# Retention of both batches in one turn, on swapped partition halves and four quarters of TensorE

## The chip, the cores and the metric

One NeuronCore of one Trainium2 chip. The metric is the device time of one execution, in microseconds (us). All five engines take part: PE (matmuls), ACT, DVE, POOL (elementwise work) and SP (which issues most of the DMAs).

## The reference

Everything is fp32. A retention (attention with a decay and without softmax) over 2 batches, 8 heads, 576 positions and 64 features a head gives x of 1152 tokens by 512. Then four experts with relu, weighted by normalized probabilities, and a second layer pair with the Mish activation.

```python
scores = (1/8) * q @ k.T                                  # per batch and head, 576 x 576
ret = scores * where(pos_i >= pos_j, gamma_h ** (pos_i - pos_j), 0)
x = (ret @ v).transpose(0, 2, 1, 3).reshape(1152, 512)
p = probs / (probs.sum(-1) + 1e-9)
y = sum(p[:, e:e+1] * (relu(x @ w1[e]) @ w2[e]) for e in range(4))   # 512 -> 1024 -> 512
h = y @ w_in                                              # 512 -> 2048
out = (h * tanh(softplus(h))) @ w_out                     # 2048 -> 512
```

## The kernel before

The retention runs in chunks of 64 positions, 9 for each batch, batch after batch, 18 in all. A chunk lies in a slot of `qkv` (6 slots of 512 KB): partitions 0-63 (`KEYS`) hold v and k by tokens, partitions 64-127 (`FEATS`) hold k and q by features. One turn on PE does three things:
- the scores of the next chunk (L434: k by features times q by features, 8 heads, contraction over 64 partitions 64-127, result on partitions 0-63 of one of three banks) interleaved head by head with the update of the state by this chunk (L438: k times decayed v, contraction over partitions 0-63, result on partitions 64-127, added up in two banks);
- at places given by `AFTER_SCORES` and `AFTER_OUTPUT`, half a tile of the first layer of expert 0 (L480 to L482; three matmuls for each product, since every fp32 operand is split into a high and a low part in fp32r);
- the output of the chunk before (L474): masked scores and state together are one operand over 128 partitions, v and q the other. DVE writes the masked scores over k (L792), so the mask has to wait until the state has been updated; ACT copies the state over k by features of the next slot (L677).

POOL multiplies v by the decay of its key (`v_decay`, L993), two chunks ahead. DVE applies the decay of the row to the output (L807), ACT and DVE split it into high and low part (L683, L813). SP loads chunks and weight blocks of 256 KB (L391, L400) in one order written out by hand. ACT makes the high part of each weight block (L354), POOL the low part (L381); a table `IN_TURN` says in which turn. The job "s" makes the sums of weight quarters that a Strassen-like product of the later stages takes (L368 to L376 on POOL, L350 on ACT).

After the retention PE takes the products of the second layer of stage 0 (`second`, 12 times three matmuls), then stage 2 and so on: 36 stages, in which first-layer products (`product`, P1 to P7) and second-layer products of the stage before alternate. Their order isn't touched. The names for the prediction: JOB "w2" u is the split of block u of the second layer; `second(1, 0)` needs block 4.

Of the kernel before, what the change touches and what calls it, by code (L numbers as in the profile page):

```python
# [13 lines left out]
P = 128  # L14
# [4 lines left out]

CH = 64  # L20
PER_BATCH = SEQ // CH
CHUNKS = BATCH * PER_BATCH
PAIRS = HEADS // 2
MID = SEQ // 2
SLOTS = 6
KEYS, FEATS = slice(0, CH), slice(CH, P)
# [9 lines left out]
PER_BLOCK = TC // CH  # L36
# [8 lines left out]
CONSTS = STEP0 + PER_BATCH * PAIRS


def has_state(c):
    return c % PER_BATCH < PER_BATCH - 1


def states(c):

    return sum(has_state(i) for i in range(c + 1))
# [3 lines left out]
TURNS = CHUNKS + 1  # L58
SCORES = 3
HS = HEADS // 2  # L60
# [3 lines left out]
AFTER_SCORES = {8: (0, 1), 9: (1, 1), 10: (2, 1), 11: (3, 1), 12: (4, 1), 13: (5, 0), 14: (5, 1),  # L64
                15: (6, 0), 16: (6, 1), 17: (7, 0), 18: (7, 1)}
AFTER_OUTPUT = {7: (0, 0), 8: (1, 0), 9: (2, 0), 10: (3, 0), 11: (4, 0)}
HIDDEN_IN = {t: c for c, (t, half) in AFTER_SCORES.items() if half}

ROWS_IN = {0: 4, 1: 5, 6: 6, 7: 7, 8: 8}
# [56 lines left out]
def plan():  # L126
# [46 lines left out]
def build(nc, chunks_in, consts_in, probs_in, weights_in, out):  # L173
    with ExitStack() as ctx:
# [5 lines left out]

        w_hi = sb("w_hi", [P, 2, UNITS, DM], F32R)
# [47 lines left out]
        mask = consts[KEYS, MASK0:ROW0]  # L229
# [4 lines left out]
        ps_s = [banks[i][KEYS, :].rearrange("p (h c) -> p h c", h=HEADS) for i in range(SCORES)]  # L234
        ps_state = [banks[i][FEATS, 0:HS * DH].rearrange("p (h c) -> p h c", h=HS) for i in range(2)]
        ps_o = banks[3][:, 0:PAIRS * CH].rearrange("p (h c) -> p h c", h=PAIRS)
# [10 lines left out]
        s_st = sem("s_st")  # L247
        s_o = sem("s_o")
# [28 lines left out]
        def by_keys(c, which):  # L277
            return qkv[KEYS, c % SLOTS, which]

        def by_feats(c, which):  # L280
            return qkv[FEATS, c % SLOTS, which]

        def landed(c):
            return 16 * (c // SLOTS + 1)

        def x_chunk(c):

            at = slice(CH * (c % PER_BLOCK), CH * (c % PER_BLOCK + 1))
            if c < PER_BLOCK:
                return x_tmp[:, c % 2], xa_hi[:, :, at], xa_lo[:, :, at]  # L290
            full = xf[:, :, CH * (c - PER_BLOCK):CH * (c - PER_BLOCK + 1)]
            if c < 2 * PER_BLOCK:
                return full, xb_hi[:, 0:KT, at], xb_lo[:, 0:KT, at]
            return full[:, KH:], xb_hi[:, KT:, at], xb_lo[:, KT:, at]
# [11 lines left out]
        def x_full(e, i):  # L306

            if e == 0:
                return (xs_a, xs_b)[i // 2][:, i % 2]
            return (x2_b[:, 0:KH], x2_c[:, KH:], x2_c[:, 0:KH], x2_b[:, KH:])[i]  # L310

# [18 lines left out]
        def weight_free(act, job):  # L330
# [56 lines left out]
        def _(sp):  # L387
            def load_chunk(c):
                if c >= SLOTS:
                    sp.wait_ge(s_o, c - SLOTS + 1)  # L390
                sp.dma_start(qkv[:, c % SLOTS], chunks_in[c]).then_inc(s_slot[c % SLOTS], 16)  # L391

            def chunk_there(c):
                sp.wait_ge(s_slot[c % SLOTS], landed(c))
# [9 lines left out]
            sp.dma_start(consts[KEYS, 0:ROW0], consts_in[KEYS, 0:ROW0]).then_inc(s_const, 16)  # L404
            load_chunk(1)

            for c in range(2, 6):
                if c > 2:
                    chunk_there(c - 3)
                load_chunk(c)  # L410
            for u in range(UNITS):
                chunk_there(3 + u)
                load_weights(u)
                chunk_there(4 + u)
                load_chunk(6 + u)
            for c in range(6 + UNITS, CHUNKS):
                chunk_there(c - 3)
                load_chunk(c)
                load_weights(UNITS + c - 6 - UNITS)
            sp.dma_start(ident[:, :], consts_in[:, CONSTS:]).then_inc(s_id, 16)  # L420
            for r in range(UNITS + CHUNKS - 6 - UNITS, len(LOADS)):
                load_weights(r)
            by_rows = out.rearrange("(g p) d -> p g d", p=P)
            sp.wait_ge(s_af, read(EXPERTS - 1, TT - 1))
            sp.dma_start(by_rows[:, 0:TT, :], acc_sb[:, 0:TT, :]).then_inc(s_out, 16)
            for g in range(TT, TPP):
                sp.wait_ge(s_af, read(EXPERTS - 1, g))
                sp.dma_start(by_rows[:, g, :], acc_sb[:, g, :]).then_inc(s_out, 16)
            sp.wait_ge(s_out, 16 * (1 + TPP - TT))

        @block.tensor
        def _(pe):
            def scores_head(c, h):
# [28 lines left out]
            def output(c):  # L462
# [7 lines left out]
                if c > 0:  # L470
                    pe.wait_ge(s_xt, c)
# [584 lines left out]
```

## Time and profile before

| | |
|---|---|
| median of 3 runs | 634.28 us (629.97 to 635.52) |
| the profiled execution | 630.54 us, span 628.8 us |
| instructions | 9476 |
| granted clock of PE over the span | 1.00 |
| DMA | 50.41 MB, mean 80 GB/s |

The span runs from the first to the last instruction of the profile. A page shows busy times by engine, a chain of work that ended last, groups of instructions, and DMA issues; the other views cut the same trace into stretches, or list it in order of time. A name in a row such as bank<-qkv is what was written and what was read.

### The profile page before, as it was taken

The page shows a single profiled execution, that of the slowest core. Times are in us where ns is not written, and L with a number is a line of the kernel's source. Part 1 is how long each engine was busy: PE and PEld are TensorE (multiplying, and loading weights), DVE is VectorE, ACT ScalarE, POOL GpSimd, SP SyncE. Part 2 cuts the span into 40 slices and gives each one's busy share as a digit, 9 for nine tenths or more (in the row PEclk, how much of TensorE's full clock was granted, in tenths as well). Part 3 has the DMA queues.
Part 4 walks back from the last instruction along what each step waited for, and adds up shares of the span by engine and source line. Part 5 has one row for each costly group of instructions (what it writes and reads, how often), then busy time and mean ns, then how long its engine had stood idle before and what let it go on. Part 6 is the DMA issues. An engine that isn't in the chain of part 4 may idle for free.

```text
span 628.8 us, 9476 instructions
## 1 busy us (share of the span) xinstructions
PE 620.6 (99%) x3764; PEld 553.7 (88%) x3765; DVE 243.5 (39%) x388; ACT 238.0 (38%) x459; POOL 284.4 (45%) x239
## 2 busy tenths in 40 slices
PE   8999999999999999999999999999999999999997
PEld 5788899998999999899999899989979999999996
DVE  5756743333143333143323143335564333314324
ACT  3555433332223432223432223435544455334432
POOL 4759535543435542535543535532553544443300
PEclk9999999999999999999999999999999999999999
DMA  8954312222112322102321202321100232201002
GB/s 275 339 177 158 111 34 68 100 88 64 51 35 67 101 84 67 51 34 67 101 84 56 62 35 67 101 67 47 55 34 34 68 116 85 68 0 52 1 0 100
DMA packets 25146, 50.41 MB, mean 80 GB/s; under 512 B 2896, under 2 KB 3216, under 8 KB 25104
## 3 DMA queue, kind: packets, MB, share of 16 engines
q1 hardware_dynamic: 24816, 49.66, 24.2%
q8 instruction: 30, 0.49, 0.3%
q10 hardware_dynamic: 288, 0.17, 0.1%
q14 instruction: 12, 0.10, 0.0%
HBM read 47.45 MB, written 2.36 MB: 79 GB/s over the span
## 4 chain that ended last, share of the span: by engine, by line
PE 95%; DVE 3%; ACT 1%; issue 0%; POOL 0%; DVEq 0%; ACTq 0%; POOLq 0%
PE bank L480 30%; PE bank L482 30%; PE bank L481 30%; PE bank L434 2%; PE bank L474 2%; DVE xt L896 1%; PE bank L612 1%; PE bank L605 1%; PE bank L438 1%; DVE acc_sb L866 0%; DVE acc_sb L870 0%; ACT h_hi L708 0%; DVE h_lo L826 0%; DVE acc_sb L975 0%; ACT h_act L691 0%
## 5 line engine op out<-in xcount | busy, mean ns | idle before, releaser
L381 POOL TENSOR_TENSOR w_lo<-w_raw,w_hi 128x512 fp32r<-128x512 f32 x96 | 128.8, 1356 | 151.0 <-ACT w_hi L354 151.0
L482 PE MATMUL bank<-w_hi,h_lo 128*128 128x512 f32 x432 | 169.9, 393 | 0.0
L481 PE MATMUL bank<-w_lo,h_hi 128*128 128x512 f32 x432 | 169.5, 392 | 0.0
L480 PE MATMUL bank<-w_hi,h_hi 128*128 128x512 f32 x432 | 169.0, 391 | 0.0
L376 POOL TENSOR_TENSOR ws<-ws_f,ws 128x1024 fp32r<-128x1024 f32 x24 | 57.9, 2412 | 150.4 <-ACT ws L350 150.4
L853 DVE TENSOR_TENSOR h_act<-part,bank 128x384 f32<-128x384 f32 x96 | 52.8, 550 | 179.4 <-PE bank L482 179.4
L482 PEld LDWEIGHTS bank<-w_hi,h_lo 128*128 128x128 f32 x432 | 81.0, 188 | 17.5
L481 PEld LDWEIGHTS bank<-w_lo,h_hi 128*128 128x128 f32 x432 | 81.0, 188 | 9.8
L480 PEld LDWEIGHTS bank<-w_hi,h_hi 128*128 128x128 f32 x432 | 81.1, 188 | 9.6
L703 ACT ACTIVATE h_hi<-h_act 128x384 fp32r<-128x384 f32 x64 | 33.6, 526 | 104.8 <-DVE h_act L853 104.8
L713 ACT ACTIVATE part<-bank 128x384 f32<-128x384 f32 x72 | 35.2, 489 | 82.9 <-PE bank L482 82.2
L480 PE MATMUL bank<-xa_hi,w_hi 128*128 128x384 f32 x192 | 66.6, 347 | 0.0
L482 PE MATMUL bank<-xa_hi,w_lo 128*128 128x384 f32 x192 | 64.7, 337 | 0.0
L481 PE MATMUL bank<-xa_lo,w_hi 128*128 128x384 f32 x192 | 64.5, 336 | 0.0
L819 DVE SCALAR_TENSOR_TENSOR h_lo<-h_act,h_hi 128x384 fp32r<-128x384 f32 x64 | 47.3, 739 | 35.5 <-ACT h_hi L703 35.5
L826 DVE TENSOR_TENSOR h_lo<-h_act,h_hi 128x384 fp32r<-128x384 f32 x48 | 32.5, 677 | 69.2 <-ACT h_hi L708 69.1
L354 ACT ACTIVATE w_hi<-w_raw 128x512 fp32r<-128x512 f32 x96 | 57.3, 618 | 0.0
L480 PE MATMUL bank<-xt,ws 128*128 128x384 f32 x144 | 48.6, 337 | 1.3 <-DVE xt L896 1.2
L481 PE MATMUL bank<-xt,ws 128*128 128x384 f32 x144 | 48.6, 337 | 0.0
L482 PE MATMUL bank<-xt,ws 128*128 128x384 f32 x144 | 48.5, 337 | 0.0
L819 DVE SCALAR_TENSOR_TENSOR h_lo<-bank,h_hi 128x384 fp32r<-128x384 f32 x32 | 17.7, 554 | 67.7 <-ACT h_hi L694 67.7
L694 ACT ACTIVATE h_hi<-bank 128x384 fp32r<-128x384 f32 x32 | 15.7, 491 | 71.2 <-PE bank L482 71.2
(87 smaller groups left out, 916.0 us busy)
## 6 DMA issues: line engine op xcount, KB each, us to landing
w_raw<-in_weights SPq DMA_DIRECT2D x144, 256.0 KB, 2.7
qkv<-in_chunks SPq DMA_DIRECT2D x18, 512.0 KB, 4.9
out<-acc_sb SPq DMA_DIRECT2D x6, 256.0 KB, 2.0
out<-acc_sb SPq DMA_DIRECT2D x1, 768.0 KB, 5.3
consts<-in_consts ACTq DMA_DIRECT2D x1, 146.0 KB, 3.8
ident<-in_consts SPq DMA_DIRECT2D x1, 64.0 KB, 4.0
consts<-in_consts SPq DMA_DIRECT2D x1, 34.0 KB, 4.0
p_nat<-in_probs ACTq DMA_DIRECT2D x1, 18.0 KB, 3.9
```

The source lines that it names most:

```text
L354: act.activation(w_hi[:, int(kind == "w2"), x], w_raw[:, r % RAW], ACT.Copy).then_inc(s_wh, 1)
L376: pool.tensor_tensor(w_sum(x)[:, 1], ws_f[:, :], w_sum(x)[:, 0].bitcast(F32), ALU.subtract)\
L381: pool.tensor_tensor(w_lo[:, layer, x], w_raw[:, r % RAW], w_hi[:, layer, x].bitcast(F32), ALU.subtract).then_inc(s_wl, 1)
L480: pe.matmul(out, w[0], x[0], start=first, stop=False, **more)
L481: pe.matmul(out, w[0], x[1], start=False, stop=False, **more)
L482: return pe.matmul(out, w[1], x[0], start=False, stop=last, **more)
L694: act.activation(h_hi[:, tile_slot(s, i)], banks[6 + i % 2][:, 0:TC], ACT.Relu).then_inc(s_hh, 1)
L703: act.activation(h_hi[:, tile_slot(s, i)], h_act[:, i % 2], ACT.Relu).then_inc(s_hh, 1)
L713: act.activation(part[:, i], banks[6][:, 0:TC], ACT.Copy).then_inc(s_pt, 1)
L819: dve.scalar_tensor_tensor(h_lo[:, slot], full, 0.0, h_hi[:, slot].bitcast(F32), ALU.max, ALU.subtract).then_inc(s_hl, 1)
L826: dve.tensor_tensor(h_lo[:, slot], h_act[:, i % 2], h_hi[:, slot].bitcast(F32), ALU.subtract)\
L853: dve.tensor_tensor(h_act[:, i % 2], part[:, kept], banks[bank][:, 0:TC], op).then_inc(s_cc, 1)
```

## The change

One turn now takes the same chunk of both batches, so there are 9 turns instead of 18 and `CH` stays 64. The two batches lie on swapped halves: batch 0 has its tokens on partitions 0-63 (`UPPER`) and its features on 64-127 (`LOWER`), batch 1 the other way. So scores of batch 0, scores of batch 1, state of batch 0 and state of batch 1 use four different quarters of the array. A slot has five columns (Y1, X0, X1, Z, Y0). The masked scores go to column Y of the batch's token half, which holds nothing loaded, and not over k, which is Z: the mask no longer waits for the state. Each slot is loaded by two transfers, one of 64 partitions for columns 0 to 3 and one of 64 partitions for columns 1 to 4. There are four slots of 1 MB; the fourth (`last_slot`) lies where `w_hi` of the second layer lies later, so its splits from block 3 on wait for the output of turn 7 (`FREE_UNITS`). Scores have two banks, the state one, the output two (before one). Tiles of the first layer are no longer cut in halves (`AHEAD`, `BEHIND`). Row decays are a ring of four instead of eight tables. The jobs of weights are spread over the turns anew; on ACT those of the last turn come behind its `first_hi`. The output is stored by two transfers, 64 partitions each, from SP (batch 0) and from ACT (batch 1).

```diff
+AHEAD = {4: 1, 5: 2, 6: 4, 7: 5, 8: 7}
+BEHIND = {3: 0, 5: 3, 7: 6}
+ROWS = 4
+ROWS_IN = {3: 5, 4: 6, 5: 7, 6: 8}
+LOW_AT_ONCE = (PER_BLOCK - 1, CHUNKS - 1)
...
     for u in range(UNITS):
-        add(IN_TURN, 5 + u, "w1", 0, u)
+        add(IN_TURN, 2 + (u + 1) // 2, "w1", 0, u)
     for u in range(3):
-        add(IN_TURN, 12 + u, "w2", 0, u)
-    add(IN_TURN, 15, "s", 0, 0)
-    for u in range(3, 6):
-        add(IN_TURN, 13 + u, "w2", 0, u)
+        add(IN_TURN, 6 + (u + 1) // 2, "w2", 0, u)
+    add(IN_TURN, 8, "w2", 0, 3)
+    add(IN_TURN, 8, "s", 0, 0)
+    for u in range(4, 6):
+        add(IN_TURN, 8, "w2", 0, u)
...
+            elif kind == "w2" and x >= FREE_UNITS:
+                act.wait_ge(s_o, CHUNKS - 1)
...
+            def load_chunk(t):
+                if t >= SLOTS:
+                    sp.wait_ge(s_o, t - SLOTS + 1)
+                sp.dma_start(slot(t)[UPPER, 0:4], chunks_in[t, UPPER]).then_inc(s_slot[t % SLOTS], 16)
+                sp.dma_start(slot(t)[LOWER, 1:5], chunks_in[t, LOWER]).then_inc(s_slot[t % SLOTS], 16)
...
+            for t in range(2, SLOTS):
+                chunk_there(t - 2)
+                load_chunk(t)
+            for t in range(SLOTS, CHUNKS):
+                chunk_there(t - 2)
+                for r in range(2 * (t - SLOTS), 2 * (t - SLOTS) + 2):
+                    load_weights(r)
+                load_chunk(t)
...
+            def scores_head(t, b, h):
+                return pe.matmul(ps_s[t % 2][FEAT[b], h], part_of(t, FEAT[b], X[b])[:, h],
+                                 part_of(t, FEAT[b], Y[b])[:, h], start=True, stop=True)
...
+            def scores_and_state(t):
+
+                n = t + 1
+                pe.wait_ge(s_slot[n % SLOTS], landed(n))
+                if n >= 2:
+                    pe.wait_ge(s_sm, BATCH * (n - 1))
+                pe.wait_ge(s_vd, BATCH * n)
+                if t > 0:
+                    pe.wait_ge(s_st, BATCH * t)
+                for h in range(HEADS):
+                    for b in range(BATCH):
+                        mm = scores_head(n, b, h)
+                    if h == HEADS - 1:
+                        mm.then_inc(s_sc, 1)
+                    for b in range(BATCH):
+                        mm = state_head(t, b, h)
+                mm.then_inc(s_kv, 1)
...
+            def first_output():
+
+                pe.wait_ge(s_vd, BATCH)
+                pe.wait_ge(s_sm, BATCH)
+                for b in range(BATCH):
+                    if b > 0:
+                        pe.wait_ge(s_of, 1)
+                    for h in range(HEADS):
+                        mm = output_head(0, b, h, TOK[b])
+                    mm.then_inc(s_o if b else s_of, 1)
+
+            def output(t):
+
+                pe.wait_ge(s_vd, BATCH * (t + 1))
+                pe.wait_ge(s_sm, BATCH * (t + 1))
+                pe.wait_ge(s_st, BATCH * t)
+                if t >= 2:
+                    pe.wait_ge(s_xt, t - 1)
                 for hp in range(PAIRS):
+                    for b in range(BATCH):
+                        for x in range(2):
+                            mm = output_head(t, b, 2 * hp + x, slice(0, P))
                 mm.then_inc(s_o, 1)
...
+            scores(0)
+            keep_warm(8)
+            for t in range(CHUNKS):
+                if t + 1 < CHUNKS:
+                    scores_and_state(t)
+                if t in AHEAD:
+                    plain_tile(AHEAD[t])
+                if t == 0:
+                    keep_warm(3)
+                    first_output()
+                else:
+                    output(t)
+                if t in BEHIND:
+                    plain_tile(BEHIND[t])
...
+            for t in range(CHUNKS):
+                if t + 1 < CHUNKS:
+                    state_copy(t)
+                if t in AHEAD:
+                    plain_hi(*divmod(AHEAD[t], ITEMS))
+                if t + 1 < CHUNKS:
+                    for job in IN_TURN.get(t, ()):
                         job_hi(act, job)
+                first_hi(t)
+                if t in BEHIND:
+                    plain_hi(*divmod(BEHIND[t], ITEMS))
+            for job in IN_TURN[CHUNKS - 1]:
+                job_hi(act, job)
...
+            def masked(t):
+
+                dve.wait_ge(s_sc, t + 1)
+                for b in range(BATCH):
+                    dve.tensor_tensor(part_of(t, TOK[b], Y[b]), ps_s[t % 2][FEAT[b]],
+                                      mask[FEAT[b]].unsqueeze(1).broadcast_to([CH, HEADS, CH]), ALU.mult).then_inc(s_sm, 1)
...
+            for t in range(CHUNKS):
+                if t + 2 < CHUNKS:
+                    v_decay(t + 2)
+                    pool.wait_ge(s_vd, BATCH * (t + 3))
+                for job in IN_TURN.get(t, ()):
                     job_lo(pool, job)
```

## Rows read from the trace of the kernel before

**Rows 1.** The page, part 1 (busy time) and part 4 (chain, shares by engine).

```profile
PE 620.6 (99%) x3764; PEld 553.7 (88%) x3765; DVE 243.5 (39%) x388; ACT 238.0 (38%) x459; POOL 284.4 (45%) x239
PE 95%; DVE 3%; ACT 1%; issue 0%; POOL 0%; DVEq 0%; ACTq 0%; POOLq 0%
```

**Rows 2.** Busy time in one stretch, the retention.

```profile
core 0: us, PE busy (x) PEld busy (x) DVE busy (x) ACT busy (x) POOL busy (x), PEclk, DMA share, GB/s
7.66:60.80 53.14, 51.01 (x917) 43.88 (x918) 34.28 (x64) 28.55 (x71) 36.96 (x33) 1.00 0.70 241
```

**Rows 3.** The same view, two stretches of 10 us.

```profile
10.00:20.00 10.00, 9.41 (x263) 8.47 (x259) 7.36 (x15) 5.15 (x15) 5.89 (x5) 1.00 0.92 314
20.00:30.00 10.00, 8.62 (x137) 7.39 (x136) 8.54 (x14) 5.31 (x13) 7.27 (x7) 1.00 0.96 342
```

**Rows 4.** The chain that ended last, by time: start us, us, what.

```profile
17.14 0.24 PE bank L434
...
18.29 0.62 PE bank L474 x16
...
20.32 1.38 issue
...
28.20 0.37 PE bank L480
28.57 0.18 PE bank L481
```

**Rows 5.** The timeline of PE at the retention's end: start us, us, instruction.

```profile
59.74 0.69 PE L474 MATMUL bank<-qkv 128*64 128x64 f32 x16
...
68.65 0.33 PE L480 MATMUL bank<-xb_hi,w_hi 128*128 128x384 f32 x1
...
69.72 0.39 PE L480 MATMUL bank<-w_hi,h_hi 128*128 128x512 f32 x1
```

**Rows 6.** The timeline of PE where blocks of two kinds overlap.

```profile
10.36 0.22 PE L474 MATMUL bank<-qkv 64*64 64x64 f32 x1
10.36 0.22 PE L438 MATMUL bank<-qkv 64*64 64x64 f32 x1
10.42 0.22 PE L434 MATMUL bank<-qkv 64*64 64x64 f32 x1
10.42 0.22 PE L474 MATMUL bank<-qkv 64*64 64x64 f32 x1
```

**Rows 7.** The page, part 6: DMA issues, KB each, us to landing.

```profile
w_raw<-in_weights SPq DMA_DIRECT2D x144, 256.0 KB, 2.7
qkv<-in_chunks SPq DMA_DIRECT2D x18, 512.0 KB, 4.9
```

**Rows 8.** The timeline of POOL: start us, us, instruction, idle before.

```profile
8.59 1.04 POOL L993 TENSOR_TENSOR qkv<-qkv,consts 64x512 f32<-64x512 f32 x1 [0.23 <-DMA qkv<-in_chunks]
9.86 1.04 POOL L993 TENSOR_TENSOR qkv<-qkv,consts 64x512 f32<-64x512 f32 x1 [0.23 <-DMA qkv<-in_chunks]
...
20.79 1.27 POOL L381 TENSOR_TENSOR w_lo<-w_raw,w_hi 128x512 fp32r<-128x512 f32 x1 [1.08 <-ACT w_hi L354]
...
54.59 0.73 POOL L368 TENSOR_TENSOR ws_f<-w_raw 128x256 f32<-128x256 f32 x1
...
58.84 2.39 POOL L376 TENSOR_TENSOR ws<-ws_f,ws 128x1024 fp32r<-128x1024 f32 x1 [1.23 <-ACT ws L350]
61.19 4.61 POOL L381 TENSOR_TENSOR w_lo<-w_raw,w_hi 128x512 fp32r<-128x512 f32 x3
```

**Rows 9.** The timeline of ACT.

```profile
8.95 0.65 ACT L677 ACTIVATE qkv<-bank 64x256 f32<-64x256 f32 x2 [6.93 <-PE bank L438]
...
57.64 1.06 ACT L350 ACTIVATE ws<-ws_f 128x1024 fp32r<-128x1024 f32 x1
```

**Rows 10.** The timeline of DVE.

```profile
8.98 0.68 DVE L792 TENSOR_TENSOR qkv<-bank,consts 64x512 f32<-64x512 f32 x1 [1.60 <-PE bank L438]
...
62.60 2.05 DVE L930 TENSOR_TENSOR xs_a<-xf 128x768 f32<-128x768 f32 x1
```

More of the change, by code:

```diff
@@ L35 @@
 KH = KT // 2
-PER_BLOCK = TC // CH
+PER_BLOCK = TC // P
 RAW = 8
 WARM = 9
-MASK0 = PER_BATCH * HEADS
+FREE_UNITS = 3
+MASK0 = CHUNKS * HEADS
 ROW0 = MASK0 + CH
 STEP0 = ROW0 + PAIRS * CH
[L45 to L69, printed above, removed]
+CONSTS = STEP0 + CHUNKS * PAIRS
+AHEAD = {4: 1, 5: 2, 6: 4, 7: 5, 8: 7}
[3 more added lines that the diff above has]
+LOW_AT_ONCE = (PER_BLOCK - 1, CHUNKS - 1)
 STAGES = 6
@@ L275, in build, with slot, part_of, landed @@
         s_out = sem("s_out")
[L277 to L292, printed above, removed]
+        def slot(t):
+            return last_slot if t % SLOTS == SLOTS - 1 else qkv[:, t % SLOTS]
+        def part_of(t, half, column):
+            return slot(t)[half, column]
+        def landed(t):
+            return 32 * (t // SLOTS + 1)
+        def x_chunk(t):
+            at = slice(P * (t % PER_BLOCK), P * (t % PER_BLOCK + 1))
+            if t < PER_BLOCK:
+                return x_tmp[:, t % 2], xa_hi[:, :, at], xa_lo[:, :, at]
+            full = xf[:, :, P * (t - PER_BLOCK):P * (t - PER_BLOCK + 1)]
+            if t < 2 * PER_BLOCK:
                 return full, xb_hi[:, 0:KT, at], xb_lo[:, 0:KT, at]
@@ L403, in _ @@
             load_chunk(0)
-            sp.dma_start(consts[KEYS, 0:ROW0], consts_in[KEYS, 0:ROW0]).then_inc(s_const, 16)
+            sp.dma_start(consts[:, 0:ROW0], consts_in[:, 0:ROW0]).then_inc(s_const, 16)
             load_chunk(1)
[L407 to L415, printed above, removed]
@@ new lines, in state_head, with scores @@
+            def state_head(t, b, h):
+                return pe.matmul(ps_state[FEAT[b], h], part_of(t, TOK[b], Z)[:, h], part_of(t, TOK[b], X[b])[:, h],
+                                 start=(t == 0 and h == 0), stop=True, skip_group_check=True)
+            def scores(t):
+                pe.wait_ge(s_slot[t % SLOTS], landed(t))
+                for h in range(HEADS):
+                    for b in range(BATCH):
+                        mm = scores_head(t, b, h)
+                mm.then_inc(s_sc, 1)
@@ L472, in output @@
+            def output(t):
[4 more added lines that the diff above has]
+                    pe.wait_ge(s_xt, t - 1)
                 for hp in range(PAIRS):
-                    for x in range(2):
-                        mm = pe.matmul(ps_o[DH * x:DH * (x + 1), hp], qkv[rows, c % SLOTS, 0, 2 * hp + x],
-                                       qkv[rows, c % SLOTS, 1, 2 * hp + x], start=True, stop=True)
+                    for b in range(BATCH):
+                        for x in range(2):
+                            mm = output_head(t, b, 2 * hp + x, slice(0, P))
@@ L907, in _ @@
             dve.wait_ge(s_rows, 16)
-            for i in range(1, 4):
+            for i in range(1, ROWS + 1):
                 rows(i)
```

260 lines of the change are left out of this document (106 added, 154 removed).

## The prediction, made before the changed kernel ran

> **What bounds the kernel now.** The page comes first. PE is busy 99% of the span and 95% of the chain that ended last is PE [rows 1]. So a change to retention is worth only what it takes out of PE's own order of work, or puts into it as waiting. The second view is the stretch of the retention, 7.66 to 60.80 us [rows 2]: PE is busy 51.01 of 53.14 us at full clock (1.00, so the upper of its two levels, 2.4 GHz), DVE 34.3, ACT 28.6, POOL 37.0, and the DMA engines 0.70. PE bounds it, and next is not an engine but the DMA: from 10 to 20 us its engines are busy 0.92 at 314 GB/s, from 20 to 30 us 0.96 at 342 GB/s [rows 3]. In these 20 us PE and the loads are nearly level. One can see that in the one long stall of PE, 1.38 us at 20.32 [rows 4]. Whatever makes PE quicker there will meet the loads.
>
> The third view is the chain in detail [rows 4]. A scores-and-state block takes 1.15 us (17.14 to 18.29), after a product 1.1. An output block of one chunk takes 0.62. A product of the first layer opens with 0.37 and then takes 0.175 for each further matmul, so half a tile (6 matmuls) is 0.37 + 5 x 0.175 = 1.24. The sum over the stretch is 17 x 1.1 + 18 x 0.62 + 16 x 1.24 = 18.7 + 11.2 + 19.8 = 49.7, and 0.6 of keep-warm products and 1.4 of stall make 51.7 of the 52.8 us up to the end of the last output at 60.4 [rows 5].
>
> **The change part by part: PE.** Each fp32 head product is two passes. In the trace of PE two passes in the same quarter start 58 ns apart (0.06 in the rows), and passes of two other quarters or lines start beside them: L474, L438 and L434 within the same 0.06 [rows 6]. So three quarters at once run at the pace of one. The new block holds scores and state of both batches, 64 passes over four quarters, 16 deep as now. If the fourth quarter is as free as the third, it costs 1.1 us, for two chunks instead of one. If PE starts passes no faster than these three in 58 ns, it costs 64 x 19.4 = 1.24 plus the 0.2 of filling; at the pace of the common two-wide stretches, 64 x 29 ns = 1.9 plus 0.2. I take 1.1, since the three-wide row is nearest, and keep 2.0 as the other end. Outputs are K=128 products on two column halves before and after: 16 passes in 0.62, so 32 passes in 0.62 + 16 x 0.028 = 1.1. The first output runs each batch by itself with a wait between, 2 x 0.62 = 1.3. Products are no longer cut in halves: 0.37 + 11 x 0.175 = 2.3 a tile. PE's new sum is 8 x 1.1 + 8 x 1.1 + 1.3 + 8 x 2.3 + 0.6 = 38 us against 51.7. By PE alone the change would gain about 14 us.
>
> Here a rule of the Trainium skill speaks against the change. "TensorE: Matmul & The Clock Gate" (section "Wait — 56ns, not 53.3ns?") says that starts of matmuls never come closer than about 25 ns however small they are. By it a block of 64 passes would be an estimated 1.6 + 0.2 us; by the rows, where three starts fit into 58 ns, the floor doesn't hold between quarters, and the sum stays.
>
> **DMA: where most of the gain goes.** The bytes are the same: 18 x 512 KB of chunks [rows 7], now 9 x 1 MB. But PE wants them sooner. Slot 0 and 1 together are the bytes of the first four chunks, and the fourth is there at 9.86, when POOL's decay of it starts [rows 8]. Today PE's first scores-and-state block starts at 7.66 with two chunks there [rows 2]; it will start at 9.9. Then each slot of 1.05 MB needs 3.4 us at 314 GB/s, and from slot 4 on two weight blocks of 256 KB go ahead of each [rows 7]: 1.57 MB, 4.6 us at 342 GB/s. The slots land at 9.9 (slot 1), 13.4, 16.7, 21.3, 25.9, 30.5, 35.1 and 39.7 (slot 8). None waits for a free slot: the load of t waits for the output of t-3, which is earlier.
>
> POOL stands between the loads and the first tiles: v_decay(t+2) is queued ahead of the splits of weights of turn t. A decay of a chunk is 1.04 us, now two a turn, 2.1; a split is 1.27 [rows 8]. Tile 0 (after output 3) needs the split that is queued behind the decay of slot 4: 21.3 + 2.1 + 1.3 = 24.7. Tile 1 needs the one behind the decay of slot 5: 25.9 + 2.1 + 1.3 = 29.3.
>
> **The turns added up.** Block 0 9.9 to 11.0, keep-warm and first output to 12.9. Block 1 waits for slot 2: 13.4, output to 15.6. Block 2 16.7, output to 18.9. Block 3 21.3, output to 23.5. Tile 0 24.7 to 27.0, block 4 to 28.1. Tile 1 29.3 to 31.6, output 32.7. From here PE doesn't wait: block 5, tile 2, output, tile 3 (1.1 + 2.3 + 1.1 + 2.3) to 39.5; block 6, tile 4, output to 44.0; block 7 starts 5 us behind slot 8, tile 5, output, tiles 6 and 7, output to 54.2. Before, it is 60.4. So 6.2 us are gained, and 7 to 8 us of PE's saving are lost to loads and POOL in the first turns.
>
> ACT and DVE have room in this. The state is copied in two pieces of twice the width: 0.65 for the pair now [rows 9], an estimated 1.1 after, against the 1.1 of the output that PE does meanwhile (up to 0.2 a turn in t = 5 to 8 if it isn't covered; only turns without a tile behind the output would show it, and there PE waits for the load). The mask costs DVE 0.68 a chunk as before [rows 10], for the turn after next. Separate places for masked scores take away the mask's wait for the state; nothing waited long for that before, and I cost it at nothing. The four row tables instead of eight and the double output bank too.
>
> **What comes behind the retention.** Here the change moves an order. The split of w2 3, the first weight sums s0 and the splits of w2 4 and 5 now stand behind the last first_hi on ACT, because w2 from 3 on lies where the last slot was. Before, s0 was begun at 54.59, six us before the retention's end, and w2 4 and 5 were done soon after it [rows 8]. Now, counted from the end of the last output: decayed 0.7, first_hi to 1.2, w2 3 on ACT to 1.8 and on POOL to 3.1; four sums of 0.73 (two DVE operations of 2.05 us beside them [rows 10] slow POOL: the three splits there took 4.61 instead of 3.8 [rows 8]) to 6.6; ACT's copy of the sums 1.06 [rows 9] to 7.7; the low part 2.39 to 10.2; w2 4 to 11.6. PE wants it when the 12 products of the second layer (8.3 us) and P1 (1.07) are through, 9.36 after the end of the output [rows 5]. So a new stall of 2.2 us; with nothing slowed it is 1.5, with all of POOL slowed by a fifth 4. Later stages have slack: the next weight sums are needed 20 us on. The output in two halves on two queues sends the same bytes; the last transfer of 128 KB instead of 256 lands no later. I cost it at 0 (bounds -0.3 to +0.5).
>
> Sum: -6.2 + 2.2 = -4.0 us. The profiled execution took 630.54 us (span 628.8), so 626.5 by its measure. The median of the runs is 634.28, 3.7 above it, so the forecast is **630.3 us**, 0.994 of before.
>
> **The rivals.** *Transfers to half of the partitions are slow.* Every load of a chunk is cut into one transfer to partitions 0-63 and one to 64-127. All loads of size in the trace go to 128 partitions, so its price isn't shown. One end is the full rate. For the other: chunks three and four land 1.26 us apart [rows 8], 415 GB/s; if that is a rate that all partitions together allow and half of them allow half, a slot takes 5.0 us, with weights 6.6. Then slot 1 lands at 13.5 and slot 8 at 56.6, and block 7, tile 5, output, tiles 6 and 7 and output (10.2 us) end at 66.8: 6.4 later than before, plus 2.2, +8.6 us, 642.9. It decides from a rate of chunk bytes below 262 GB/s (slot 8 at 48.0). For it speaks that the transfers of one slot run one behind the other; against it that several are in flight and may fill each other's gaps, which would leave it between.
> The Trainium skill, "SBUF — State Buffer" (sections "Door 1: The DMA port swizzle" and "Can I just issue two DMAs to hit both halves?"), says that partitions 0-63 reach only half of the ports, and that two transfers to the two halves serialize, only 6% better than one. By its 218 GB/s the estimate would be +6.3 us. No row here shows it.
>
> *The four quarters don't run at once.* Blocks of 2.0 us: in t = 4 to 7 nothing hides the 0.9, +3.6; 633.9 and no gain.
>
> *No stall behind the retention.* If POOL gets through in time or the loads come earlier than I count them (10% faster loads are 1.5 us at tile 1), it is -6 to -8: 627.5.
>
> **How the numbers follow.** A measurement of this kernel can't tell less than about 1% (6.3 us) from no change. The forecast has 0.44, with its own bounds from 626 to 634: 0.05 of it under 628, the rest same. Slow half transfers 0.33, 635 to 643: 0.21 slower by over 1%, 0.12 same. No overlap of quarters 0.08, all same. No stall 0.15, 0.11 faster. Together faster 0.16, same 0.63, slower 0.21. The range holds the forecast and most of both sides, 625 to 643.
>
> **What the profile would show.** The timeline of PE: blocks of 64 passes of 1.1 us, or 2.0. The waits: POOL's qkv for DMA, with slot 8 there near 40, or near 55. The DMA share in the first 30 us stays at 0.9 and over in all cases, but the GB/s stay at 330 or fall to about 210. PE idle for w_lo of the second layer some 9 us behind the retention. The clock stays 1.00: if the waits of up to 2.4 us in turns 1 to 3 bring it down to 1.2 GHz, the blocks double in length there, yet mostly inside waits for loads. The forecast is wrong if PE waits for slots 6 to 8, or if the last output ends before 52 or after 57.

## The result, and the profile after

The changed kernel takes 653.76 us (median of 4 runs, 652.6 to 654.02), the one before 633.07 (4 runs, 629.97 to 635.52): ratio 1.033, with an interval of 1.029 to 1.036. It is slower, by about 21 us. The profiled execution has a span of 652.1 us against 628.8, so 23.3 us are to be found in the two traces.

The page of the changed kernel, parts 1 (busy time), 4 (shares of the chain that ended last) and 6 (DMA issues):

```profile
PE 621.4 (95%) x3768; PEld 554.8 (85%) x3768; DVE 244.4 (37%) x370; ACT 235.1 (36%) x434; POOL 288.7 (44%) x239
...
PE 84%; DMA 9%; DVE 2%; POOL 2%; issue 1%; ACT 1%; SPq 1%; POOLq 0%
...
qkv<-in_chunks SPq DMA_DIRECT2D x14, 512.0 KB, 10.1
out<-acc_sb SPq DMA_DIRECT2D x6, 128.0 KB, 2.4
out<-acc_sb ACTq DMA_DIRECT2D x6, 128.0 KB, 2.9
```

Beside [rows 1]: PE's share of the chain fell from 95% to 84%, and DMA now has 9%. A transfer of 512 KB of a chunk takes 10.1 us from issue to landing, against 4.9 [rows 7].

The same kernel's busy time in stretches (stretch and length in us; then busy us and instructions of PE, PEld, DVE, ACT, POOL; the granted clock of PE; the mean busy share of the DMA engines; GB/s):

```profile
5.00:15.00 10.00, 5.73 (x105) 3.61 (x104) 2.81 (x6) 0.00 (x0) 3.02 (x3) 0.83 1.04 223
15.00:45.00 30.00, 20.23 (x423) 17.78 (x413) 16.08 (x21) 10.48 (x18) 13.66 (x13) 0.74 1.03 231
65.00:70.00 5.00, 5.00 (x32) 4.56 (x34) 0.96 (x2) 0.96 (x3) 1.65 (x2) 0.50 0.36 108
```

The first two lines are the result in short: they are the stretches in which the slots are loaded. The DMA engines are as busy as in [rows 3] (1.03 against 0.92 and 0.96), but move 223 and 231 GB/s instead of 314 and 342. A share of 1.0 looks like a full pipe; only the GB/s beside it show that it isn't. PE is busy two thirds of the time from 15 to 45 us, at a clock between its levels (0.74).

The timeline of POOL shows when slots land: before each decay of v shown here it stood idle, and the load ended the idle time (in brackets).

```profile
14.05 2.15 POOL L1026 TENSOR_TENSOR qkv<-qkv,consts 64x512 f32<-64x512 f32 x2 [2.71 <-DMA qkv<-in_chunks]
18.91 2.15 POOL L1026 TENSOR_TENSOR qkv<-qkv,consts 64x512 f32<-64x512 f32 x2 [2.70 <-DMA qkv<-in_chunks]
...
54.24 2.15 POOL L1026 TENSOR_TENSOR last_slot<-last_slot,consts 64x512 f32<-64x512 f32 x2 [2.41 <-DMA last_slot<-in_chunks]
...
61.74 2.15 POOL L1026 TENSOR_TENSOR qkv<-qkv,consts 64x512 f32<-64x512 f32 x2 [2.73 <-DMA qkv<-in_chunks]
...
77.93 1.87 POOL L393 TENSOR_TENSOR w_lo<-w_raw,w_hi 128x512 fp32r<-128x512 f32 x1 [5.28 <-ACT w_hi L366]
79.76 1.46 POOL L380 TENSOR_TENSOR ws_f<-w_raw 128x256 f32<-128x256 f32 x1
...
84.13 0.75 POOL L385 TENSOR_TENSOR ws_f<-w_raw,ws_f 128x256 f32<-128x256 f32 x1
86.11 2.36 POOL L388 TENSOR_TENSOR ws<-ws_f,ws 128x1024 fp32r<-128x1024 f32 x1 [1.23 <-ACT ws L362]
88.43 7.86 POOL L393 TENSOR_TENSOR w_lo<-w_raw,w_hi 128x512 fp32r<-128x512 f32 x4
```

Slot 1 is there at 14.05, slot 2 at 18.91 and slot 8 at 61.74. Between slot 1 and 2 it is 4.86 us for 1.05 MB, 216 GB/s; between slot 7 and 8 it is 7.50 us for 1.57 MB with its weight blocks, 210 GB/s. So the blocks of weights, transfers to all 128 partitions, go no faster when they stand between half transfers.

The timeline of PE, around slot 8 and behind the retention:

```profile
61.72 0.27 PE L441 MATMUL bank<-qkv 64*64 64x64 f32 x2 [1.93 <-DMA qkv<-in_chunks]
61.73 0.27 PE L445 MATMUL bank<-last_slot 64*64 64x64 f32 x2
...
61.88 0.22 PE L441 MATMUL bank<-qkv 64*64 64x64 f32 x2
61.89 0.23 PE L445 MATMUL bank<-last_slot 64*64 64x64 f32 x2
61.94 0.23 PE L441 MATMUL bank<-qkv 64*64 64x64 f32 x2
61.95 0.23 PE L445 MATMUL bank<-last_slot 64*64 64x64 f32 x2
...
62.64 0.23 PE L441 MATMUL bank<-qkv 64*64 64x64 f32 x2
...
64.82 0.66 PE L505 MATMUL bank<-xa_hi,w_hi 128*128 128x384 f32 x1 [1.94 <-issue]
...
74.92 1.15 PE L476 MATMUL bank<-qkv 128*64 128x64 f32 x32
...
90.47 0.71 PE L505 MATMUL bank<-w_hi,h_hi 128*128 128x512 f32 x1 [4.95 <-POOL w_lo L393]
```

The four quarters do what the change says: L441 and L445 start two passes each (x2), and the next four start 58 ns later, where [rows 6] has three. The block of 64 passes for two chunks runs from 61.72 to 62.88, in 1.16 us. An output of 32 passes takes 1.15. What is gained there is lost again in PE's waits for the loads, 12.1 us in all up to the retention's end (the kernel before has none).

Where the 23.3 us went:
- The last output ends at 76.0 instead of 60.4 [rows 5]: +15.6. Slot 8 comes at 61.7, and the rest takes 14.3 us.
- PE waits 4.95 us for block 4 of the second layer, a wait that the kernel before hasn't.
- Behind that wait PE runs at the lower clock for some microseconds (0.65 from 90 to 92 us, its matmuls 0.43 us apart instead of 0.23), +1.8 (stage 2's first matmul of P6 begins at 95.96 instead of 73.53, 22.4 us later, and 15.6 + 5.0 of these are in the two points above).
- The end: from DVE's last add to the end of the span 3.4 us instead of 2.5, +0.9.

### The profile page after: what moved, and what is told of

Its sections match the earlier page's. It is cut to its first block, busy times and chain, and to the rows that moved or that the text cites. A ratio compares the mean times of both kernels' runs of the same rounds, so it can differ in the third digit from the quotient of the medians.

```text
span 652.1 us, 9388 instructions
## 1 busy us (share of the span) xinstructions
PE 621.4 (95%) x3768; PEld 554.8 (85%) x3768; DVE 244.4 (37%) x370; ACT 235.1 (36%) x434; POOL 288.7 (44%) x239
## 4 chain that ended last, share of the span: by engine, by line
PE 84%; DMA 9%; DVE 2%; POOL 2%; issue 1%; ACT 1%; SPq 1%; POOLq 0%
PE bank L506 28%; PE bank L507 28%; PE bank L505 28%; DMA qkv<-in_chunks 9%; POOL w_lo L393 1%; DVE xt L922 1%; PE bank L628 1%; SPq L403 0%; POOL ws L388 0%; SPq L413 0%; DVE acc_sb L892 0%; DVE acc_sb L896 0%; DVE h_lo L852 0%; DVE acc_sb L1004 0%; POOL ws_f L381 0%
## 5 line engine op out<-in xcount | busy, mean ns | idle before, releaser
L393 POOL TENSOR_TENSOR w_lo<-w_raw,w_hi 128x512 fp32r<-128x512 f32 x96 | 131.7, 1388 | 144.0 <-ACT w_hi L366 143.6
L507 PEld LDWEIGHTS bank<-w_hi,h_lo 128*128 128x128 f32 x432 | 81.3, 188 | 17.6
L507 PE MATMUL bank<-xa_hi,w_lo 128*128 128x384 f32 x192 | 66.2, 345 | 0.0
L506 PE MATMUL bank<-xa_lo,w_hi 128*128 128x384 f32 x192 | 66.0, 344 | 0.0
## 6 DMA issues: line engine op xcount, KB each, us to landing
qkv<-in_chunks SPq DMA_DIRECT2D x14, 512.0 KB, 10.1
last_slot<-in_chunks SPq DMA_DIRECT2D x4, 512.0 KB, 10.2
```

Of the source, the lines that this page charges most:

```text
L393: pool.tensor_tensor(w_lo[:, layer, x], w_raw[:, r % RAW], w_hi[:, layer, x].bitcast(F32), ALU.subtract).then_inc(s_wl, 1)
L506: pe.matmul(out, w[0], x[1], start=False, stop=False, **more)
L507: return pe.matmul(out, w[1], x[0], start=False, stop=last, **more)
```

## The experiments

Unless it says otherwise, an experiment changes one thing in the kernel before or in the changed kernel ("after"). Ratios are to the kernel before on the same chip, with their 95% interval.

**1. The kernel before with its chunks cut into halves by partitions.**

```diff
-sp.dma_start(qkv[:, c % SLOTS], chunks_in[c])
+sp.dma_start(qkv[KEYS, c % SLOTS], chunks_in[c, KEYS])      # 0-63
+sp.dma_start(qkv[FEATS, c % SLOTS], chunks_in[c, FEATS])    # 64-127
```

> The kernel before, with every 512 KB load of a chunk cut into a transfer to partitions 0-63 and one to 64-127; nothing else. Theory (a transfer to half of the partitions runs at about 215 GB/s): a chunk takes 2.4 us to load instead of 1.5, with a weight block 3.2 to 3.8. The turns without a product (1.8 us) wait for it, those with a tile (4.2 us) don't: 5 x 0.6 + 3 x 1.6, some 8 us slower, 6 to 10, and 210 to 240 GB/s in the first 25 us. Rival (the number of transfers or their issue costs it): the same loss as in the run cut by columns. Rival (layout of slots, chain of waits or array of the changed kernel costs it): no change, 0 to 1 us.

Measured: 637.45 us against 632.52, ratio 1.007 (1.005 to 1.010). The same bytes and the same order, and 4.9 us more. Window, and the timeline of POOL:

```profile
3.00:15.00 12.00, 11.13 (x142) 6.84 (x140) 3.94 (x11) 1.72 (x5) 4.14 (x4) 1.00 1.05 235
```

```profile
10.86 1.04 POOL L994 TENSOR_TENSOR qkv<-qkv,consts 64x512 f32<-64x512 f32 x1 [1.27 <-DMA qkv<-in_chunks]
13.16 1.04 POOL L994 TENSOR_TENSOR qkv<-qkv,consts 64x512 f32<-64x512 f32 x1 [1.26 <-DMA qkv<-in_chunks]
```

A chunk takes 2.3 us (10.86 to 13.16) instead of the 1.27 of [rows 8], 228 GB/s, with the DMA engines at 1.05. The price was expected too high, at 8 us (6 to 10): the kernel before wants a chunk only every 2.9 us on average, and PE's waits for chunks add up to 2.9 us.

**2. The same with two transfers cut by columns**, each to all 128 partitions.

```diff
+for w in range(2):
+    sp.dma_start(qkv[:, c % SLOTS, w], chunks_in[c, :, w])
```

> The kernel before, with every load of a chunk cut into two transfers of 256 KB that both go to all 128 partitions (v or k by features, then k or q). Theory: no change, within 1 us, and 310 to 340 GB/s in the first 25 us. Rival (number of transfers): as slow as the run cut by partition halves.

Measured: 633.67 against 632.52, 1.002 (0.999 to 1.005): no difference. Window of this kernel:

```profile
5.00:10.00 5.00, 5.00 (x32) 2.96 (x33) 0.67 (x3) 0.00 (x0) 3.01 (x3) 1.00 0.97 341
```

Twice the transfers, half as large, at 341 GB/s. From 10 to 15 us it is 232 GB/s, but there the DMA engines are busy only 0.70 of the time, so that isn't a low rate of the transfers. So neither the number nor the size of the transfers is at fault.

**3. The changed kernel with one transfer a slot**, to all partitions. A slot has five columns of which each half needs four, so the fifth is sent as zeros: 1.31 MB instead of 1.05.

```diff
-sp.dma_start(slot(t)[UPPER, 0:4], chunks_in[t, UPPER])
-sp.dma_start(slot(t)[LOWER, 1:5], chunks_in[t, LOWER])
+sp.dma_start(slot(t)[:, :], chunks_in[t])
```

> The changed kernel, with each slot loaded by one transfer to 128 partitions of all five columns. It carries a column of zeros in each half that nobody reads: 1.31 MB a slot instead of 1.05. Theory: at 320 to 340 GB/s a slot takes 3.9 us, with weights 5.5: slot 1 near 12, slot 8 near 47 instead of 61.7; last output near 58 instead of 76, and some 15 to 18 us faster than the changed kernel in spite of 25% more bytes (636 to 639). The wait for the second layer's w2 4 (5 us) stays. Rival (the array or the waits of the turn hold it up, not the loads): not over 3 us faster, or slower by the added bytes.

Measured: 636.13 against 632.52, 1.004 (1.002 to 1.006); 17.6 us less than the changed kernel's median, with a quarter more bytes. Its windows, and its timeline of PE:

```profile
5.00:15.00 10.00, 7.49 (x207) 5.17 (x208) 7.10 (x14) 1.81 (x3) 5.50 (x6) 1.00 0.99 395
15.00:45.00 30.00, 23.92 (x532) 21.74 (x533) 18.84 (x28) 15.10 (x27) 19.93 (x18) 0.89 0.94 346
```

```profile
25.18 0.37 PE L440 MATMUL bank<-qkv 64*64 64x64 f32 x2 [3.52 <-DMA qkv<-in_chunks]
...
56.55 1.15 PE L475 MATMUL bank<-qkv 128*64 128x64 f32 x32
...
72.10 0.80 PE L504 MATMUL bank<-w_hi,h_hi 128*128 128x512 f32 x1 [4.95 <-POOL w_lo L393]
```

POOL begins the decay of slot 8 at 45.86 instead of 61.74 (it comes to it from other work, so the slot is there by then at the latest), and the last output ends at 57.7, before the 60.4 of [rows 5]. Yet the kernel isn't faster: the wait for w2 4 (the split of block 4 of the second layer) stands unchanged, 4.95 us. Loads cost the change its gain, and the order of POOL's jobs costs it the rest.

**4. The changed kernel with the lower halves issued by ACT**, the upper ones by SP, so that two queues work side by side.

```diff
 sp.dma_start(slot(t)[UPPER, 0:4], chunks_in[t, UPPER])
-sp.dma_start(slot(t)[LOWER, 1:5], chunks_in[t, LOWER])
+# on ACT, for t < 4 at the start, else behind first_hi(t - 4)
+act.dma_start(slot(t)[LOWER, 1:5], chunks_in[t, LOWER])
```

> The changed kernel, with the half transfers to partitions 64-127 issued by ACT instead of SP, so that both halves are in flight on two queues at the same time. Theory A (the two queues' transfers mix on the DMA engines and so reach all partitions at once): over 300 GB/s, as fast as with one transfer, 12 us or more faster than the changed kernel. Theory B (the halves hinder each other as much from two queues): within 2 us of the changed kernel, at 215 to 230 GB/s.

Measured: 652.81 against 632.52, 1.031 (1.026 to 1.035), as the changed kernel. Window of this kernel:

```profile
10.00:15.00 5.00, 5.00 (x60) 2.86 (x62) 1.38 (x2) 0.00 (x0) 3.25 (x4) 1.00 1.02 231
```

Still 231 GB/s, and slot 8 at 61.73. Two queues gain nothing over one. This agrees with the Trainium skill, "SBUF — State Buffer" (section "Can I just issue two DMAs to hit both halves?"), which says that transfers issued from several engines run on the same DMA engines, and that two transfers to the two halves serialize.

**5. One transfer a slot, and the first weight sums s0 a turn earlier** (in turn 7, ahead of the splits of w2 1 and 2).

```diff
-add(IN_TURN, 8, "s", 0, 0)
+add(IN_TURN, 7, "s", 0, 0)    # w2 0 to turn 6, w2 1 and 2 behind s0
```

> The kernel with one transfer a slot, with the weight sums s0 moved in the table of jobs from turn 8 to turn 7, ahead of the splits of w2 1 and 2 (so on POOL they come before the retention's end and not behind the last first_hi). Theory (the order of jobs makes the wait of PE for w2 4 behind the retention): the wait of 5.0 us goes, and with it the half clock behind it (1.8 us): 6 to 7 us faster than with one transfer alone, 629 to 631. Rival (POOL is full there, whatever the order): another split or the sums are late in its place, the wait stays over 3 us.

Measured: 628.58 against 631.87, 0.995 (0.993 to 0.998). By the ratios that is 0.9 points (5.6 us) below 3, where 6 to 7 us were expected. The wait for w2 4 is gone, with the last output at 58.4, 0.7 us later than in 3. The view of waits of this kernel, for PE (engine, line, releaser: us in total, times, longest):

```profile
PE bank L441 <- DMA qkv<-in_chunks: 5.0, 3, 3.1
```

**6 and 7. What makes a half slow: 64 partitions, or these 64?** The kernel before with three transfers a chunk: once 0-31, 32-95, 96-127, once 0-31, 32-63, 64-127.

```diff
+for rows in (slice(0, 32), slice(32, 96), slice(96, 128)):    # 6
+for rows in (slice(0, 32), slice(32, 64), slice(64, 128)):    # 7
+    sp.dma_start(qkv[rows, c % SLOTS], chunks_in[c, rows])
```

> The kernel before, with each load of a chunk cut into three transfers: partitions 0-31, 32-95 and 96-127. Theory A (what counts is whether a transfer has partitions of both halves, below and from 64): the middle transfer, half of the bytes, runs at the full rate, the outer two at 215 GB/s: 2.0 us a chunk, 260 GB/s in the first 15 us. Theory B (64 or 32 partitions are slow as such, few rows for 16 DMA engines): no faster than with 0-31, 32-63, 64-127, about 215 to 240 GB/s.

> The kernel before, with the same three sizes cut otherwise: partitions 0-31, 32-63 and 64-127, so that no transfer has partitions of both halves. Both theories: 2.4 us a chunk, 215 to 240 GB/s, as the run cut in halves. It stands beside the run with 0-31, 32-95, 96-127.

Measured: 638.19 (1.010, 1.007 to 1.014) and 638.09 (1.010, 1.006 to 1.013) against 631.87. Windows, first of the kernel with 32-95, then of the other:

```profile
3.00:15.00 12.00, 10.37 (x148) 6.73 (x148) 4.97 (x12) 1.72 (x5) 4.15 (x4) 0.86 1.00 225
```

```profile
3.00:15.00 12.00, 11.44 (x154) 7.15 (x154) 4.72 (x14) 1.93 (x6) 4.14 (x4) 1.00 1.04 234
```

A chunk takes 2.44 us with the middle piece in one and 2.29 without. If a transfer that takes partitions of both halves ran at the full rate, as the theory of the halves has it, the first would be at 2.0. So this pair speaks against that theory, or else the two outer pieces of 32 partitions, one in each half, cost more than their bytes. The pair can't tell which; 9, 13 and 14 look at it in other ways.

**8. The kernel before with its stores in two halves**, from SP and from ACT, as the change has them.

```diff
-sp.dma_start(out, acc_sb)
+sp.dma_start(by_rows[KEYS, ...], acc_sb[KEYS, ...])
+act.dma_start(by_rows[FEATS, ...], acc_sb[FEATS, ...])
```

> The kernel before, with each store of the result cut into partitions 0-63 from SP and 64-127 from ACT, as in the changed kernel; nothing else. Theory (the split of the store costs the 0.9 us that the tail of the changed kernel is longer, from the last DVE row to the end of the span): 0.9 us more, the tail 3.4 instead of 2.5 us. Rival (the store's rows lie apart in DRAM in the changed kernel, and that costs it): tail 2.5 as before.

Measured: 633.56 against 631.87, 1.002 (1.000 to 1.004). The page, part 6, and the timeline of DVE of this kernel:

```profile
out<-acc_sb ACTq DMA_DIRECT2D x6, 128.0 KB, 2.9
```

```profile
624.23 2.05 DVE L872 TENSOR_TENSOR acc_sb<-bank,acc_sb 128x512 f32<-128x512 f32 x3 [2.03 <-PE bank L482]
```

The last add ends at 626.3 as before, and the span at 629.7 instead of 628.8. The tail of 3.4 us is that of the changed kernel: the 0.9 us come from the store. In the times this size can't be told from nothing.

**9. The kernel before with its chunks cut into even and odd partitions**: 64 partitions a transfer, but spread over all 128.

```diff
+for i in range(2):
+    sp.dma_start(qkv[i::2, c % SLOTS], chunks_in[c, i::2])
```

> The kernel before, with each load of a chunk cut into its even and its odd partitions (64 each, spread over both halves). Theory A (a transfer that takes one half of the partitions is slow because of which half): full rate, 310 to 340 GB/s in the first 15 us, 1.5 us a chunk and within 2 us of the kernel before. Theory B (any transfer to 64 partitions is slow): 215 to 240 GB/s, 2.4 us a chunk, some 5 us slower. The run with 32-95 spoke for B.

Measured: 632.86 against 632.74, 1.000 (0.997 to 1.002). Window of this kernel:

```profile
3.00:15.00 12.00, 11.62 (x205) 8.05 (x204) 6.60 (x14) 2.89 (x9) 5.57 (x6) 1.00 0.92 305
```

305 GB/s where the halves have 235 in the same stretch, and a chunk every 1.3 us. The same bytes in two transfers of 64 partitions each: what is slow is not any 64 partitions. The 64 of one half are.

**10. The changed kernel with only s0 a turn earlier**, its half transfers kept.

> The changed kernel as it is (half transfers), with the sums s0 moved from turn 8 to turn 7, ahead of the splits of w2 1 and 2. Theory: the wait of 5.0 us for w2 4 and the half clock behind it go here too, 5 to 7 us faster than the changed kernel, 646 to 648; the rest, over 13 us, is the loads'. Rival (the wait only shows once the loads are quick): no change.

Measured: 644.28 against 632.74, 1.017 (1.013 to 1.021), 9.5 us less than the changed kernel, where 5 to 7 were expected. The wait of 5.0 and the lower clock behind it (1.8) are gone, as counted. What wasn't counted is that the last output ends at 74.1, 1.9 earlier (slot 8 lands 1.1 earlier, at 60.64; no run shows why): together 8.7 (the spans differ by 8.3).

**11. The kernel of 5 without the loads of turns 4 to 8**: POOL and PE use what lies in the slots, so the results of these turns are not the reference's. It shows what faster loads of these turns could give at most.

```diff
+if t >= SLOTS:
+    return    # in load_chunk
```

> The kernel with one transfer a slot and the sums early, in which the loads of turns 4 to 8 are left out: the four slots are loaded once and used again, so the result isn't the reference's; POOL waits for the output that read the slot. It shows the turns without their loads. Theory (four quarters and fewer turns save PE about 14 us, and loads eat it): the last output ends near 48 to 50 instead of 58, 8 to 10 us faster than the kernel with the sums early. Rival (the turn itself, its chain of decay, split, mask and state copy, is what lasts): not over 3 us faster.

Measured: 625.29 against 632.74, 0.987 (0.982 to 0.992). By the ratios that is 0.8 points (5 us) below the kernel of 5; 8 to 10 us were expected. Timeline of PE of this kernel:

```profile
19.51 0.92 PE L475 MATMUL bank<-qkv 128*64 128x64 f32 x23 [3.55 <-issue]
...
53.95 1.15 PE L475 MATMUL bank<-qkv 128*64 128x64 f32 x32
```

From 19.5 on PE waits only once more (0.57 us at 27.20, for DVE), with its clock at 0.66 from 20 to 25 us, and the last output ends at 55.1, where 48 to 50 was expected. That is 0.9 us later than the 54.2 that the prediction gave for loads at full rate. The first four slots and all blocks of weights are still loaded here, and the wait of 3.55 us lies among them, so it isn't shown what loads without any price would give. Without those of turns 4 to 8 the change gains 1.3%.

**12. The kernel of 5 with the load of slot 4 ahead of its two weight blocks.**

```diff
+if t == SLOTS:
+    load_chunk(t)    # then load_weights twice
```

> The kernel with one transfer a slot and the sums early, in which slot 4 is loaded ahead of the first two weight blocks instead of behind them. Theory: PE's wait of 3.1 us for slot 4 shrinks by the 1.4 us of 512 KB, and tile 0, which needs a split of the first block, comes no later: 0.5 to 1.5 us faster than with the sums early, 627 to 628. Rival (the wait only moves to w1 0 and 1): no change within 0.5 us.

Measured: 627.82 against 632.74, 0.991 (0.988 to 0.994): faster than both kernels, with the lowest median of the complete ones, though its interval overlaps that of 5 (0.993 to 0.998). It is 2.5 us above the kernel of 11, which was timed beside it. Window and waits of PE:

```profile
20.00:25.00 5.00, 2.62 (x104) 2.31 (x102) 4.08 (x6) 2.80 (x5) 3.85 (x4) 1.00 1.05 418
```

```profile
PE bank L444 <- DMA qkv<-in_chunks: 1.8, 2, 1.1
PE bank L479 <- issue: 2.6, 1, 2.6
PE bank L448 <- issue: 2.7, 2, 1.7
```

PE waits for loads 1.8 us instead of the 5.2 of 5, but 5.6 us in all in "issue" (a row of 0.3 is left out) instead of 3.6. The last output ends at 56.2 instead of 58.4. So the wait for slot 4 went, and part of it came back in other waits.

**13 and 14. One extra transfer of 196 KB behind chunks 0, 1, 3 and 4 of the kernel before**, to buffers that nobody reads yet: once to partitions 0-63, once to 32-95. Each chunk stays one transfer to 128 partitions. Each kernel ran once, so only the traces are read, not the times.

```diff
+sp.dma_start(spare[0:64, 0:768], ...)     # 13
+sp.dma_start(spare[32:96, 0:768], ...)    # 14
```

> The kernel before, with one more transfer of 196 KB behind each load of chunks 0, 1, 3 and 4, to partitions 0-63 of a place that is free then; its data is not used. Both theories: each adds 0.9 us at 215 GB/s, so POOL's decay of the sixth chunk (13.57 in the kernel before) comes some 3.6 us later.

> The same, with the added transfers to partitions 32-95, which take 32 partitions of each half. Theory A (slow is what stays in one half, so this one is not slow, and in the run cut at 32 and 96 the outer pieces did the harm): each adds 0.5 us, the sixth chunk's decay some 2 us later than in the kernel before. Theory C (an unbroken run of 64 partitions is slow wherever it lies, and only even and odd ones or all 128 are not): 3.6 us later, like the run with 0-63.

Measured: 635.93 and 631.59 against 631.62. Windows, first with 0-63, then with 32-95; then the timeline of POOL of each, the sixth chunk's decay last:

```profile
3.00:12.00 9.00, 8.23 (x63) 4.27 (x64) 2.38 (x8) 0.63 (x2) 3.39 (x3) 1.00 1.03 319
```

```profile
3.00:12.00 9.00, 7.78 (x124) 5.12 (x125) 5.23 (x12) 1.30 (x4) 3.96 (x4) 1.00 1.00 367
```

```profile
12.56 1.03 POOL L997 TENSOR_TENSOR qkv<-qkv,consts 64x512 f32<-64x512 f32 x1 [1.49 <-DMA ws_f<-in_chunks]
15.07 1.04 POOL L997 TENSOR_TENSOR qkv<-qkv,consts 64x512 f32<-64x512 f32 x1 [1.48 <-DMA h_act<-in_chunks]
16.34 1.03 POOL L997 TENSOR_TENSOR qkv<-qkv,consts 64x512 f32<-64x512 f32 x1 [0.23 <-DMA qkv<-in_chunks]
```

```profile
11.27 1.04 POOL L997 TENSOR_TENSOR qkv<-qkv,consts 64x512 f32<-64x512 f32 x1 [0.67 <-DMA ws_f<-in_chunks]
13.01 1.04 POOL L997 TENSOR_TENSOR qkv<-qkv,consts 64x512 f32<-64x512 f32 x1 [0.71 <-DMA h_act<-in_chunks]
14.30 1.04 POOL L997 TENSOR_TENSOR qkv<-qkv,consts 64x512 f32<-64x512 f32 x1 [0.25 <-DMA qkv<-in_chunks]
```

With 0-63 the sixth chunk comes at 16.34, 2.8 us later than in the kernel before (13.57), where 3.6 was expected; with 32-95 it comes at 14.30, 0.7 later, where the theories had 2 and 3.6. The sixth chunk, which has no extra, takes 1.27 us in the first and 1.29 in the second. The one ahead of it, with an extra, takes 2.51 in the first (12.56 to 15.07), so 196 KB to 0-63 cost 1.24 us, 159 GB/s; in the second it takes 1.74 (11.27 to 13.01) and the one ahead of that 1.77, so the same bytes to 32-95 cost some 0.47 us, about 418 GB/s. So beside transfers to all partitions, 64 neighbouring partitions are fast if they lie across the middle, and slow if they lie in one half.

Experiment 6 isn't explained by that. If its middle piece of 262 KB went at 418 GB/s, it took an estimated 0.6 us, and 1.8 are left for the two others of 131 KB each, 146 GB/s. But in 7 three pieces, two of them of that size, took 2.29 us for the 524 KB of a chunk, 229 GB/s, so a piece of 32 partitions isn't that slow as such. Whether in 6 the middle piece was slow between the outer ones, or these were slow with one in each half, no run tells.

## Why the prediction was wrong

**The step that failed is "the slots land at full rate".** The forecast put them at 9.9 (slot 1) to 39.7 (slot 8), at 314 and 342 GB/s. They landed at 14.05 to 61.74, at 216 and 210. Nothing else has such a size: with one transfer to all partitions (experiment 3) 17.6 us come back although more bytes are sent, and cutting alone brings 228 GB/s to the kernel before (experiment 1), while other cuts into two (2 and 9) cost nothing. The argument against this rival, that several transfers in flight may fill each other's gaps, is refuted by 1 and 4. The rule of the Trainium skill that was named with it, in "SBUF — State Buffer", is borne out: its 218 GB/s stands beside 210 to 235 here. The estimate of +6.3 us that was worked out from it is smaller still than the rival's own +8.6, and fell short with it.

**The rival named the mechanism but gave 66.8 for the last output and 642.9 in all.** The measured 653.76 lies above it, and above the whole range of 625 to 643. Five of its terms were too small. For each of the first slots it had 5.0 us, and 4.9 to 5.9 was measured. With weight blocks it had 6.6, pricing them at the full rate of [rows 3], and 6.8 to 7.8 was measured: they share the low rate. That is slot 8 at 61.7 instead of 56.6, 5.1 us. From slot 8 to the end it had 10.2, and 14.3 was measured: PE stands 1.94 us in "issue" at 64.82, the 12 matmuls of tile 5 and the output behind it run at the lower clock (0.50 from 65 to 70 us, matmuls 0.32 apart instead of 0.18), +2.2. The stall behind the retention was 2.8 more than its 2.2, the lower clock behind it 1.8, the store 0.9. 5.1 + 4.1 + 2.8 + 1.8 + 0.9 = 14.7, which with the rival's 8.6 makes the 23.3.

**The prices of PE's own work were right**, as were POOL's decay (2.15 for 2.1) and the DMA share that stays at 1.0 while the GB/s fall. Four quarters at once: 1.16 us for a block against 1.1, output 1.15 against 1.1, and no floor between starts of different quarters. The rival of quarters one after the other is out. In experiment 11 PE works from 19.5 to 55.1 us, 35.6; by the forecast's prices the same blocks, outputs and tiles are 33.5, and 0.57 of waiting and the lower clock from 20 to 25 us are to be added. One reading was wrong: the "about 14 us" set 38 us of work against 51.7, which hold the stall of 1.4; without it the saving is about 12. That stall itself (20.32 in [rows 4]) is put down to "issue" and not to a load, so it didn't show that PE and the loads are level; the waits for loads in 3 and 5 do. In the three complete kernels with one transfer a slot (3, 5, 12) the retention ends at 57.7, 58.4 and 56.2: of the 12 us 2 to 4 arrive there, where the forecast had 6.2.

**The stall behind the retention was seen in the right place and mis-sized.** 2.2 us was forecast, with an end of 4 if all of POOL were slowed by a fifth; it is 4.95. The forecast gave the four sums 3.5 us, 0.73 each and 0.6 more for DVE's work beside them; they took 5.1. Three of them took about 1.46, and the split of w2 3 took 1.87 instead of 1.27, while DVE ran operations with two inputs, of which these two are also longer than the 0.95 of one ahead of them:

```profile
80.54 1.50 DVE L962 TENSOR_TENSOR xs_a<-xf,xs_a 128x768 f32<-128x768 f32 x1
82.07 1.39 DVE L964 TENSOR_TENSOR xs_b<-xs_a,xf 128x768 f32<-128x768 f32 x1
```

The fourth sum (84.13), with DVE idle, took 0.75. First_hi ended 1.3 us behind the output where 1.2 was counted, so the chain didn't begin late; it is POOL's speed. In 5, where the sums stand a turn earlier, they take 1.00 once and 0.74 three times. Experiments 5 and 10 show that the order of jobs makes this a wait of PE: with s0 a turn earlier it is gone, and no other wait of its size comes in its place. In 3, where the loads were right, the stall is worth 0.9 points or 5.6 us by the ratios of 3 and 5: the difference between a time that is slightly slower and one that is slightly faster.

**The clock.** The forecast said that waits might bring it down inside other waits only. It fell to 0.74 from 15 to 45 us, which lies mostly inside waits for loads, as said, but the stretches behind slot 8 and behind the wait for w2 4 were on the path: about 2.2 + 1.8 us.

**The store** was costed at nothing with 0.5 as the upper end; in the traces of 8 and of the changed kernel it is 0.9 us. The half sent by ACT's queue takes 2.9 us to land instead of 2.4. The median of 8 is 1.7 above, with an interval that just holds no change.

Open stays why the kernels with good loads don't get all of it. "Issue" is 3.6 us of PE's waiting up to 130 us in 5 and 5.6 in 12. In the changed kernel and in 3, 4, 5, 10, 11 and 12 one such wait stands at the same matmul, behind the ninth pass of turn 1's output, with 1.24, 1.15, 4.35, 1.48, 2.37, 3.55 and 2.58 us. The DMA engines needn't be full for it: in 11 their share is 0.88 from 16 to 18 us and 0.21 from 18 to 19.5. The view of DMA shows a transfer on the instruction queue inside this wait in 11 (between 17 and 18 us) and 12 (between 15 and 16), and just before it in 5 (between 14 and 15). It may be that PE's instructions come late behind the loads. No run separates this from other causes.

## What to carry to other kernels

Read the GB/s beside the busy share of the DMA engines: 1.03 with 230 GB/s is a pipe at two thirds. When a layout swaps halves of the partitions, keep its load one transfer over all 128 partitions, even if that sends a quarter more bytes; if it must be cut, cut by columns or into even and odd partitions. And when a phase gets shorter or its steps merge, list the jobs that were hidden in it and what waits for them: here moving one job by a turn was worth 5.6 us in one kernel and 9.5 in another.

## What was not expected of the hardware

- Four quarters of the array start four fp32 passes in 58 ns, as three do [rows 6].
- One transfer of 10 KB a partition ran at 395 to 418 GB/s in stretches (experiments 3 and 12; 346 from 15 to 45 us in 3), above the 314 to 342 of the kernel before with 4 KB [rows 3].
- Blocks to all partitions that are queued among transfers to one half share their low rate: 1.57 MB in 7.5 us, a third of it such blocks. If the halves take the 4.86 us that they take alone, an estimated 2.6 are left for 0.52 MB, 199 GB/s.
- POOL's sums of 128x256 took 1.46 us beside DVE's two-input operations and 0.75 with DVE idle, and a split 1.87 instead of 1.27.
- PE stood in "issue" for 1.2 to 4.4 us at one and the same matmul in the middle of an output block, in all kernels with the new turns; its cause is open.
